# A second buffer for output rows and their places, and expert numbers named ahead of rows, in the expert stage of a fused RWKV + dense MLP + top-1 MoE kernel

## What is computed

```python
logits = x @ w_gate                         # x: 3072 x 384, w_gate: 384 x 8
e_idx = argmax(logits, axis=1)
gate_w = softmax(logits)[arange(N), e_idx]
eom = 1 / (1 + exp(-(x @ w_output_gate)))
for e in range(8):
    mask = e_idx == e
    h = maximum(x[mask] @ w1[e], 0.0)       # w1[e]: 384 x 1024
    ye = h @ w2[e]                          # w2[e]: 1024 x 384
    out[mask] = gate_w[mask, None] * eom[mask, e, None] * ye
```

## Time and profile before

| | us |
|---|---|
| median of 3 runs | 887.0 (886.81 to 889.1) |
| the profiled execution | 887.55 |
| its span in the trace | 885.7 |
| rest of it, outside the span | 1.85 |

### The profile page before, as it was taken

One profiled execution on the slowest core, in us unless ns is written; L12 is line 12 of the kernel. 1 busy time (PEld: TensorE's weight loads), 2 busy tenths in 40 slices (PEclk: granted clock), 3 DMA queues, 4 the chain that ended last, 5 costly groups with the idle time before them and its releaser, 6 DMA issues.

```text
span 885.7 us, 15606 instructions
## 1 busy us (share of the span) xinstructions
PE 851.0 (96%) x5725; PEld 759.2 (86%) x5725; DVE 570.2 (64%) x1045; ACT 316.5 (36%) x503; POOL 182.4 (21%) x145
## 2 busy tenths in 40 slices
PE   5799999999999999999999999999699999999996
PEld 4688888888888888888888888899699999999995
DVE  8778756675568546543444446467778778977771
ACT  1233223111311131112211221356176766777661
POOL 4923202232123403140101001003112111011110
PEclk9999999999999999999999999999799999999999
DMA  9843420242024402340010002547397778766700
GB/s 380 285 162 132 132 105 13 83 153 83 0 64 128 135 1 65 100 130 1 11 45 36 1 1 80 208 180 238 144 415 258 260 278 302 263 237 252 286 17 19
DMA packets 35935, 125.79 MB, mean 142 GB/s; under 512 B 4044, under 2 KB 19328, under 8 KB 30256
## 3 DMA queue, kind: packets, MB, share of 16 engines
q1 hardware_dynamic: 31504, 108.20, 34.4%
q0 software_dynamic: 3520, 9.87, 2.9%
q10 hardware_dynamic: 864, 7.08, 2.2%
HBM read 107.32 MB, written 18.88 MB: 142 GB/s over the span
## 4 chain that ended last, share of the span: by engine, by line
PE 91%; DVE 3%; DMA 3%; issue 2%; POOL 1%; ACT 0%; POOLq 0%; DVEq 0%
PE bank L1525 33%; PE bank L1569 6%; PE bank L1571 6%; PE bank L1570 6%; PE bank L1622 4%; PE bank L1620 4%; PE bank L1621 4%; PE bank L1601 4%; PE bank L1602 3%; PE bank L1603 3%; PE bank L1598 3%; PE bank L1450 3%; PE bank L1470 2%; PE bank L1435 2%; PE bank L1462 2%
## 5 line engine op out<-in xcount | busy, mean ns | idle before, releaser
L1525 PE MATMUL bank<-X1H,WH 128*128 128x512 f32 x432 | 169.5, 392 | 4.2 <-DVE X1L L1040 4.2
L1525 PE MATMUL bank<-X1H,WL 128*128 128x512 f32 x432 | 168.9, 391 | 0.0
L1525 PE MATMUL bank<-X1L,WH 128*128 128x512 f32 x432 | 168.7, 390 | 0.0
L1186 DVE TENSOR_TENSOR TT<-bank,SG 128x512 f32<-128x512 f32 x72 | 49.7, 691 | 120.5 <-ACT SG L764 120.0
L764 ACT ACTIVATE SG<-bank 128x512 f32<-128x512 f32 x72 | 43.0, 598 | 234.6 <-PE bank L1525 229.9
L694 ACT ACTIVATE AH<-PP 128x512 fp32r<-128x512 f32 (+1 forms) x78 | 46.2, 599 | 162.3 <-DVE PP L1191 162.3
L1525 PEld LDWEIGHTS bank<-X1H,WH 128*128 128x128 f32 x432 | 81.5, 189 | 21.1 <-issue 4.3
L1525 PEld LDWEIGHTS bank<-X1H,WL 128*128 128x128 f32 x432 | 81.4, 188 | 17.1
L1194 DVE TENSOR_TENSOR AL<-PP,AH 128x512 fp32r<-128x512 f32 (+1 forms) x78 | 63.2, 817 | 50.9 <-ACT AH L694 49.4
L1525 PEld LDWEIGHTS bank<-X1L,WH 128*128 128x128 f32 x432 | 81.6, 189 | 16.7
L1569 PE MATMUL bank<-AH,WH 128*128 128x512 f32 (+1 forms) x234 | 91.0, 389 | 0.0
(11 more groups left out here) (225 smaller groups left out, 1859.6 us busy)
## 6 DMA issues: line engine op xcount, KB each, us to landing
W_EVEN<-w SPq DMA_DIRECT2D x20, 1536.0 KB, 9.1
W_ODD<-w SPq DMA_DIRECT2D x18, 1536.0 KB, 7.7
RK_IN<-unit_rk SPq DMA_DIRECT2D x18, 736.0 KB, 5.6
V_IN<-unit_v SPq DMA_DIRECT2D x18, 448.0 KB, 3.8
STG<-w_dense ACTq DMA_DIRECT2D x6, 1152.0 KB, 5.9
X<-mixed SPq DMA_DIRECT2D x6, 768.0 KB, 4.4
mixed<-YS SPq DMA_DIRECT2D x40, 96.0 KB, 2.0
XG_ODD<-store SPq DMA_DIRECT2D x9, 394.0 KB, 8.5
```

Source lines behind the costliest of these rows:

```text
L1186: tt(TT[:, :], GATE_PS[:, :], SG[:, :], ALU.mult).then_inc(gate_free, 1)
L1525: last = mm(bank_[:, :], lhs[:, f, m, k * P:k * P + P], rhs[:, k, :], start=(x == 0), stop=(x == len(terms) - 1))
```

## The change

`YO` and `IDX` get a second buffer, chosen by the tile's parity, and `out_written` becomes two semaphores, one for each buffer. A new number of each tile, `of_buffer`, counts the halves that earlier tiles of the same buffer send; `set_index` waits for those alone. `plan_rows` loses the three steps that give the expert numbers; they become `plan_experts`, which stands right behind `plan_entries` and announces itself with `experts_ready`. SP waits for that, starts w1 and w2 of tile 3, then waits for `plan_ready` and the rest as before and starts tile 3's rows; w1, w2 and rows of tile 4 follow. The number of instructions on each engine stays what it was. The new `YO` takes the place of `X1` and `X2T` (dense stage), half of which the old one took.

```diff
-    YO = place(list(d), "YO", [P, 2, DM])
+    YO = place(list(d), "YO", [P, 2, 2, DM])
-    IDX = place(e_, "IDX", [P, 2], I32)
+    IDX = place(e_, "IDX", [P, 2, 2], I32)
...
-    EARLY_TILES = [ExpertTile(t, 2 * t, 2 * t - 2, 2, t % 2, t // 2) for t in range(EARLY)]
+    EARLY_TILES = [ExpertTile(t, 2 * t, 2 * t - 2, t // 2 * 2, 2, t % 2, t // 2) for t in range(EARLY)]
...
+            first, second = late_tiles(0)
+            sp.wait_ge(experts_ready, 1)
+            sp.nop(nofuse=True)
+            load_weights(first, late_expert(0))
             sp.wait_ge(plan_ready, 1)
             sp.wait_ge(records_sent, 1 + CH)
             sp.wait_ge(pad_written, 16 * NE)
             sp.nop(nofuse=True)
-            for place_, tile in enumerate(late_tiles(0)):
-                load_tile(tile, late_row(place_), late_expert(place_), place_ == 0)
+            load_rows_when_free(first, late_row(0))
+            load_tile(second, late_row(1), late_expert(1))
...
                     nc.gpsimd.indirect_dma_start(
-                        out=out[:, :], out_offset=bass.IndirectOffsetOnAxis(ap=IDX[:, half:half + 1], axis=0),
-                        in_=YO[:, half, :], in_offset=None, bounds_check=TOK - 1, oob_is_err=False)\
-                      .then_inc(out_written, 16)
+                        out=out[:, :], out_offset=bass.IndirectOffsetOnAxis(ap=IDX[:, tile.buffer, half:half + 1], axis=0),
+                        in_=YO[:, tile.buffer, half, :], in_offset=None, bounds_check=TOK - 1, oob_is_err=False)\
+                      .then_inc(out_written[tile.buffer], 16)
...
             def set_index(tile):
-                need(dve, out_written, 16 * tile.before)
+                need(dve, out_written[tile.buffer], 16 * tile.of_buffer)
                 dve.wait_ge(scale_ready, tile.n + 1)
                 rows_ = slice(0, len(tile.halves))
-                nc.vector.tensor_copy(IDX[:, rows_], IDF[:, rows_]).then_inc(index_ready, 1)
+                nc.vector.tensor_copy(IDX[:, tile.buffer, rows_], IDF[:, rows_]).then_inc(index_ready, 1)
...
+            def plan_experts(q):
+                q.step(tt(TA[:, :, :], TB[:, :, :], by_entry(CST[:, C_EXP:C_EXP + 2 * NE], both), ALU.mult))
+                q.step(nc.vector.tensor_reduce(ETF[:, :], TA[:, :, :], AX.X, ALU.add))
+                nc.vector.tensor_copy(ETI[:, :], ETF[:, :]).then_inc(experts_ready, 1)
+
             def plan_rows(q):
...
                 q.step(nc.vector.tensor_reduce(STF[:, :], TA[:, :, :], AX.X, ALU.add))
-                q.step(tt(TB[:, :, :], TB[:, :, :], by_entry(CST[:, C_EXP:C_EXP + 2 * NE], both), ALU.mult))
-                q.step(nc.vector.tensor_reduce(ETF[:, :], TB[:, :, :], AX.X, ALU.add))
-                nc.vector.tensor_copy(ETI[:, :], ETF[:, :])
                 nc.vector.tensor_copy(STI[:, :], STF[:, :]).then_inc(plan_ready, 1)
...
             set_index(tile)
             plan_entries(plan)
+            plan_experts(plan)
             w1_lows(following, (0,))
             x_lows(following)
             w1_lows(following, (1, 2))
             plan_rows(plan)
```

More of the change, by code:

```diff
@@ L221, in rwkv_moe_moe, with __init__ @@
     class ExpertTile:
-        def __init__(self, n, before, two_before, halves, buffer, nth_load, nth_half_tile=None):
+        def __init__(self, n, before, two_before, of_buffer, halves, buffer, nth_load, nth_half_tile=None):
             self.n, self.before, self.halves, self.buffer = n, before, range(halves), buffer
-            self.two_before = two_before
+            self.two_before, self.of_buffer = two_before, of_buffer
             self.loaded = 16 * nth_load + 16
@@ L231, in __init__ @@
             self.after = before + halves
-    EARLY_TILES = [ExpertTile(t, 2 * t, 2 * t - 2, 2, t % 2, t // 2) for t in range(EARLY)]
-    END_TILES = [ExpertTile(TILES - 2, HALVES - 4, HALVES - 5, 2, 1, TILES // 2 - 1),
-                 ExpertTile(TILES - 1, HALVES - 2, HALVES - 4, 2, 0, TILES // 2)]
+    EARLY_TILES = [ExpertTile(t, 2 * t, 2 * t - 2, t // 2 * 2, 2, t % 2, t // 2) for t in range(EARLY)]
+    END_TILES = [ExpertTile(TILES - 2, HALVES - 4, HALVES - 5, 2 + 2 * LATE_HALVES, 2, 1, TILES // 2 - 1),
+                 ExpertTile(TILES - 1, HALVES - 2, HALVES - 4, 4 + LATE_HALVES, 2, 0, TILES // 2)]
     def late_tiles(i):
-        return (ExpertTile(EARLY + 2 * i, 2 * EARLY + 3 * i, 2 * EARLY + 3 * i - 1, 2, 1, i + 1),
-                ExpertTile(EARLY + 2 * i + 1, 2 * EARLY + 3 * i + 2, 2 * EARLY + 3 * i, 1, 0, i + 2, i))
+        return (ExpertTile(EARLY + 2 * i, 2 * EARLY + 3 * i, 2 * EARLY + 3 * i - 1, 2 + 2 * i, 2, 1, i + 1),
+                ExpertTile(EARLY + 2 * i + 1, 2 * EARLY + 3 * i + 2, 2 * EARLY + 3 * i, 4 + i, 1, 0, i + 2, i))
     class Unit:
@@ L374, in rwkv_moe_moe @@
         base_ready = sem("base_ready")
+        experts_ready = sem("experts_ready")
         plan_ready = sem("plan_ready")
@@ L399, in rwkv_moe_moe @@
         index_ready = sem("index_ready")
-        out_written = sem("out_written")
+        out_written = [sem(f"out_written{i}") for i in range(2)]
         block = ctx.enter_context(nc.Block())
@@ L514, in late_expert, with load_weights @@
                 return sp.value_load(ETI[0:1, bass.ds(i, 1)], min_val=0, max_val=NE - 1)
[L516 to L522, removed]
+            def load_weights(tile, e):
                 sp.wait_ge(w1_low, 3 * tile.n - 3)
@@ L528, in load_tile, with load_rows_when_free @@
                 load_w2(e, tile.buffer)
[L529 to L534, removed]
+            def load_rows_when_free(tile, row):
+                sp.wait_ge(scale_ready, tile.n - 1)
+                sp.nop(nofuse=True)
+                sp.wait_ge(x_turned, tile.two_before)
+                sp.nop(nofuse=True)
+                load_rows(tile, row)
+            def load_tile(tile, row, e):
+                load_weights(tile, e)
+                load_rows_when_free(tile, row)
             sp.wait_ge(r_scaled, UNITS)
@@ L686, in _ @@
                 send_outputs(tile)
-            pool.wait_ge(out_written, 16 * HALVES)
+            for last in END_TILES:
+                pool.wait_ge(out_written[last.buffer], 16 * (last.of_buffer + 2))
             pool.nop(nofuse=True)
@@ L843, in scale_rows @@
                     act.wait_ge(yo_ready, tile.before + half + 1)
-                    nc.scalar.activation(YO[:, half, :], YO_PS[half][:, 0:DM], ACT.Copy,
+                    nc.scalar.activation(YO[:, tile.buffer, half, :], YO_PS[half][:, 0:DM], ACT.Copy,
                                          scale=SC[:, tile.buffer, half:half + 1]).then_inc(yo_scaled, 1)
```

## The result

The changed kernel takes 883.43 us, the median of 5 runs (881.6 to 885.01). Runs of the kernel before beside them gave 888.98 us (886.81 to 889.1). The ratio is 0.9945, with a 95% interval of 0.9922 to 0.9968, so the change gains 4.9 us (2.8 to 6.9). The forecast was a gain of 8.8 us and 878.2 us, in a range that ended at 881.2. The direction was right, the size was not, and the time lies outside the range.

What follows compares the result with a forecast made beforehand. From 588 us PE's products bound the kernel, plus two waits (7.6 and 0.4 us) and clock losses. Terms: 6.68 + 2.88 - 1.0 + 0.2 = 8.8 us, from 887.0 to 878.2 us; 8-in-10 range 876.8 to 881.2.

Steps and rivals of the forecast that it cites:

- DVE's wait before tile 1's cast goes: At tile 1's set_index: second buffers remove the wait for tile 0's output; PE starts tile 2 6.68 us earlier, moved steps included.
- clock whole in tile 2's up products: At tile 2's expert_up: after a gap of 0.89 us the clock stays full, 8.16 us instead of 11.04, gaining 2.88 us.
- w1's start to the rows' landing: Tile 3's transfers on SP's queue: w1 starts at 620.1 and the rows, behind both weights, land at 632.3.
- later tiles: After tile 3: casts wait for outputs two tiles back instead of one; 0.2 us gained, bounds 0 and 0.4.
- the cost of the moved steps: On DVE before tile 2's low parts: two steps and a cast for expert numbers delay PE's tile 2 by 1.00 us.
- the cover of tile 3's weights on ACT and DVE: Before tile 3's products: its weights are split by 638.1, ahead of PE at 641.3, so nothing there is late.
- part 3: Tile 3's loads: rows queued behind both weights land at 632.3, PE wants them at 631.32; a new wait of 1.0 us.
- Tile 3's weights queue behind the last pads, till about 622: On SP's queue: the pads end about 622; w2 lands 9.4 us later at 631.4, the rows 0.9 us behind it.
- The term's own upper bound: PE's wait for tile 3's rows: tile 1's two output blocks beside the weights can add 0.9 us, making it 1.9.
- the forecast's nearest row: Clock after PE's pauses: it stayed at 1.00 after a gap of 1.14 us, taken as nearest to the 0.89 us left.
- the rows come much later: Rival at tile 3's rows: 2 to 6 us of wait; at the pads' pace 5.3 us, time 882.7 to 885.6; chance 0.15.

Runs made afterwards that it cites:

- again: The changed kernel run once more, unaltered, on one chip with three variants, against the kernel before: ratio 0.9947 (0.9931 to 0.9963).
- The buffers alone: Against the kernel before: second output buffers only; expert numbers stay behind tile 2's low parts, tile 3's rows load ahead of its weights. Ratio 0.9885.
- the plan alone: Against the kernel before: expert numbers and tile 3's weights early, but one buffer for output rows and places. Ratio 1.0005 (0.999 to 1.0021).

## Why the prediction was wrong

| step | forecast | measured in the trace |
|---|---|---|
| DVE's wait before tile 1's cast goes, PE starts tile 2 sooner | 6.68 us | 6.85 (24.90 to 18.05 from tile 1's first product) |
| left of PE's gap before tile 2 | 0.9 | 0.7 |
| clock whole in tile 2's up products | 2.88 gained | gained, PEclk 1.00 |
| the pads have landed | 622 | 626.1, again 629.8 (624.0 and 627.3 with the later starts taken off) |
| w1's start to the rows' landing | 12.2 | 14.7, again 15.7 |
| PE's wait for the rows | 1.0 | 3.1, again 4.5 |
| clock behind this wait | whole | fell, 1.64 lost |
| later tiles | 0.2 gained | 0.3 gained (235.8 to 235.5 from tile 3's first product to the end) |
| the start of the kernel | 0 | 2.12 later in this execution |

**Right**: what the buffers bring, the time at which the pads had landed in the kernel before (622, and 622.3 by SP's wait), the cost of the moved steps, the cover of tile 3's weights on ACT and DVE, and the place of the new wait. The buffers alone show it purely: 44.94 us, less the whole gap of 7.57, less 2.88 of slow products, plus the new wait of 1.4, is 35.9, and 35.91 was measured.

**Wrong, and decisive**: the size of one term in part 3, "at **632.3**", and with it the new wait of 1.0 us. The mechanism was there, rows that queue behind 3 MB of weights, but from w1's start to the rows' landing it took 14.7 and 15.7 us and not 12.2, and PE waited 3.1 and 4.5 us. Two steps of that sum failed.

First, "Tile 3's weights queue behind the last pads, till about 622" took an end that was right for the old trace over to the new kernel. There the pads had landed at 626.1 and 629.8, or 624.0 and 627.3 with the later starts of 2.12 and 2.53 us taken off, 2 and 5 us behind the forecast.

Second, the 12.2 us from w1's start to the rows' landing, meant for a queue that is still busy with pads, are what a nearly idle queue needs. With the plan alone, in the same order and with the pads long landed, it was 12.4 us, and the kernel before took 12.7 for the same three transfers in its order (634.76 to 647.4, behind a DMA share of 0.01). With the pads landed before w1's start, but four output blocks sent around it, it was 13.5; with all pads and a quarter of the outputs of tiles 0 and 1, 14.1; with all of both, 14.7 and 15.7. The term's own upper bound, 1.9 us of wait, took in half of the outputs that ran beside the weights, those of tile 1 and not those of tile 0.

How the miss divides between pads and outputs is not shown. By the traces, moving half of the pads took more off the wait (3.1 and 4.5 to 1.6) than leaving out three quarters of these outputs (to 2.2); by the times it is the other way round (0.9913 and 0.989). The record of the semaphores shows what a late end looks like: a DMA announces its landing by 16 increments, and for w1 in the changed kernel 15 of them come from 628.70 to 629.62 and the last at 631.15, for the rows 14 up to 635.14 and two at 636.39 and 636.64. A small part of these transfers lands some 1.5 us behind the rest, in the kernel before too (w1: 15 up to 642.03, the last at 643.90).

**The second miss** follows from it. At 1.0 us of pause the clock would have stayed, and the forecast's nearest row was right for that. The runs fill the distance that it had left open: whole after 1.6 and 1.7 us, fallen after 2.2, 2.3, 3.1 and 4.5.

**What was weighed wrongly**: the rival "the rows come much later" had the mechanism, and had 0.15. With the waits and the fall measured, its sum comes out: 6.68 + 2.88 + 0.2 - 3.1 - 1.64 = 5.0 us, and 4.9 were gained. The rival's own wait was 5.3 us, though, from the pads' pace, and its gain 1.4 to 4.3. That the measured 883.4 lies in its 882.7 to 885.6 is luck, as the base was 2 us low. The ring-order rule of the Trainium skill ("DMA: Bandwidth & Descriptors", section "Queues, rings and completion order") spoke for it: on each DMA engine the rows stand behind the weights. It was used to set the term at 1.0 us, but the runs show the price of this order: with the rows first no wait at all, with both weights first 3.1 and 4.5 us. That the second part of the change could be worth less than nothing was not among the rivals. Undoing it brings the ratio from 0.9947 to 0.9899, and with the experts' steps moved back too it was 0.9885.

**The base** was the third miss: the forecast subtracted from a median of three runs, which was 2 us low.

## What to carry to other kernels

When a load is moved ahead, ask what now stands behind it in its queue, and which of the two is wanted first: here the small rows (394 KB) were wanted before 3 MB of weights. Give the first-wanted transfer the front, or split the large one around it: w1, rows, w2 took the stage from 40.3 to 35.3 us, and leaving the order as it was, with the second buffers alone, to 35.9 at the same time. And when a block of transfers is moved, compare the sum for it with its length from first start to last landing in the old trace: here that was 12.7 us with an idle queue, and the sum had 12.2 with a busy one. The time at which a queue was free in the old trace need not hold in the new kernel.

## What the runs showed of the hardware

The start of the kernel differs between executions in which the same instructions run. The same 16 products, in the trace of the kernel before and in that of the changed one:

```profile
18.45 1.09 PE L1470 MATMUL bank<-AM,V_START 128*64 128x128 f32 x16
```

```profile
19.00 1.97 PE L1478 MATMUL bank<-AM,V_START 128*64 128x128 f32 x16
```

They took 1.8 times as long, and the products behind them too, and at tile 1's first product the new trace was 2.1 us behind. That is near the ratio of the clock's two levels. The view gives 1.00 there in both traces, but the record of the granted clock only begins at 17.92 us in the kernel before and at 22.72 in the changed one, both times with 1.00; with the buffers alone, also a fast start, it begins at 16.63. So the products are slow until this first entry, and that the clock is at its lower level till then is inferred. The kernel before varies as well (886.0 to 892.3 over all its runs), and half of a gain of 5 us can hide in it: distances inside the trace told the experiments apart where times could not.

The clock fell after pauses from 2.2 us on and stayed after pauses up to 1.7, where the kernel before had only 1.14 and 4.25 to go by, and 24 products without use, put into such a wait, kept it at 2.4 GHz and gave back 1.6 us between the turned rows and tile 3's first product.
